# Gates of the first MoE split by halves of the tokens, its second chunk's sums prepared inside the first chunk, and the first places and orders of the second MoE changed

## What is computed

```python
def _attn_ref(q, k, v, tau):                     # 4 x 8 heads, 576 x 64
    scores = scale * q @ k.T
    scores = where(scores >= max(scores) - tau, scores, -1e9)
    return softmax(scores) @ v
def _moe_ref(x, w_a, w_b, w_out):                # x 2304 x 512, w_a and w_b 512 x 1536
    return ((x @ w_a) * (x @ w_b)) @ w_out
def _moe2_ref(x, w_in, w_out, g_ln):             # w_in 512 x 1024
    h = x @ w_in
    solu = h * softmax(h)
    return (layer_norm(solu) * g_ln) @ w_out
```

## Time and profile before

| what | value |
|---|---|
| runs | 976.65, 977.17, 977.37 us; median 977.17 |
| profiled execution | 976.68 us, of which the span from first to last instruction is 974.6 us |
| attention | to about 328 us |
| chunk 0 of the first MoE | about 328 to 378.7 us |
| chunks 1 to 4 | 378.7 to about 757 us, 95.0 us each for the middle ones |
| second MoE | from about 757 us |
| granted TensorE clock | 0.998 of full speed over the span |

### The profile page before, as it was taken

How to read it: one execution, slowest core, us unless ns; L and a number is a source line. 1 busy time by engine, 2 the same in 40 slices (tenths; PEclk the granted TensorE clock), 3 DMA queues, 4 the chain that set the end, 5 groups by cost and what they waited for, 6 DMA issues and landing times.

```text
span 974.6 us, 18670 instructions
## 1 busy us (share of the span) xinstructions
PE 943.8 (97%) x6222; PEld 869.4 (89%) x6222; DVE 779.4 (80%) x1298; ACT 508.6 (52%) x823; POOL 601.4 (62%) x570
## 2 busy tenths in 40 slices
PE   5999999999999998999999999999999999999998
PEld 5999999999998998999899999998899778888886
DVE  6778778887878577787878787877888888888884
ACT  3777777777778645333533443335434743333332
POOL 2777777777778454666576657665777754433320
PEclk9999999999999999999999999999999999999999
DMA  6666667666674564222322231123220200000001
GB/s 176 167 153 164 162 151 169 160 152 161 155 176 112 155 213 131 83 69 67 87 87 66 66 108 65 65 73 143 66 76 13 87 23 22 22 22 22 22 22 43
DMA packets 55683, 96.76 MB, mean 99 GB/s; under 512 B 15576, under 2 KB 24408, under 8 KB 55632
## 3 DMA queue, kind: packets, MB, share of 16 engines
q1 hardware_dynamic: 55632, 96.10, 35.9%
HBM read 58.41 MB, written 5.32 MB: 65 GB/s over the span
## 4 chain that ended last, share of the span: by engine, by line
PE 55%; issue 17%; POOL 13%; DVE 8%; ACT 2%; DMA 2%; SPq 1%; POOLq 0%; DVEq 0%; ACTq 0%
PE PS L1678 12%; PE PS L1640 9%; PE PS L1642 8%; POOL w_raw L739 4%; POOL w_raw L736 3%; PE PS L1837 3%; PE PS L1838 3%; PE PS L1839 3%; POOL w_raw L730 3%; PE PS L1894 3%; PE PS L1896 3%; PE PS L1895 3%; POOL w_raw L738 2%; PE PS L1705 2%; PE PS L1707 2%
## 5 line engine op out<-in xcount | busy, mean ns | idle before, releaser
L664 POOL TENSOR_TENSOR p_lo<-prob,p_hi 128x576 fp32r<-128x576 f32 x144 | 208.6, 1451 | 49.8 <-ACT p_hi L859 47.8
L1705 PE MATMUL PS<-x_parts,w_parts 128*128 128x256 f32 x672 | 191.8, 285 | 8.1 <-DVE g_parts L1332 4.2
L1640 PE MATMUL PS<-ops 128*128 128x288 f32 x642 | 182.1, 305 | 13.8 <-DVE ops L1287 6.5
L1706 PE MATMUL PS<-x_parts,w_parts 128*128 128x256 f32 x672 | 190.8, 284 | 0.0
L1707 PE MATMUL PS<-x_parts,w_parts 128*128 128x256 f32 x672 | 190.8, 284 | 0.0
L1642 PE MATMUL PS<-ops 128*128 128x288 f32 x642 | 177.5, 298 | 0.0
L1207 DVE TENSOR_REDUCE neg_max<-PS 128x1 f32<-128x576 f32 x144 | 108.5, 755 | 59.5 <-PE PS L1642 59.4
L732 POOL TENSOR_TENSOR w_parts<-w_raw,w_parts 128x768 fp32r<-128x768 f32 x48 | 90.8, 1893 | 92.4 <-ACT w_parts L986 92.4
L1640 PEld LDWEIGHTS PS<-ops 128*128 128x128 f32 x642 | 122.5, 191 | 22.7 <-issue 12.0
L1705 PEld LDWEIGHTS PS<-x_parts,w_parts 128*128 128x128 f32 x672 | 129.5, 193 | 12.2 <-DVE g_parts L1332 5.7
L1706 PEld LDWEIGHTS PS<-x_parts,w_parts 128*128 128x128 f32 x672 | 129.5, 193 | 1.8
(11 more groups left out here) (170 smaller groups left out, 2271.1 us busy)
## 6 DMA issues: line engine op xcount, KB each, us to landing
w_raw<-w_ab_dram SPq DMA_DIRECT2D x60, 512.0 KB, 3.3
qk_raw<-qkT_dram SPq DMA_DIRECT2D x32, 288.0 KB, 3.0
ops<-qk_hi SPq DMA_DIRECT2D x62, 144.0 KB
ops<-qk_hi SPq DMA_DIRECT2D x31, 288.0 KB
ops<-qk_lo SPq DMA_DIRECT2D x62, 144.0 KB
v_raw<-v_tiles_dram SPq DMA_DIRECT2D x32, 160.0 KB, 2.7
xT<-head_sb SPq DMA_DIRECT2D x32, 144.0 KB, 3.1
out_dram<-o_sb SPq DMA_DIRECT2D x18, 256.0 KB, 2.0
```

The costliest lines, as they stand in the source:

```text
L664: pool.tensor_tensor(p_lo[:, s, :], prob[:, s, :], p_hi[:, r, :].bitcast(F32), ALU.subtract).then_inc(p_lo_done, 1)
L1640: pe.matmul(ps[:, b, 0:HALF], weights[0][:, r, own], moving[0][:, r, cols], start=(n == 0), stop=False)
L1705: pe.matmul(up_ps(bank, half), w[:, 0, :], x[:, 0, :], start=(k == 0), stop=False)
L1706: pe.matmul(up_ps(bank, half), w[:, 0, :], x[:, 1, :], start=False, stop=False)
```

## The change

- The gates of chunks 1 to 4 are split by halves of the tokens. The first gate is put into the second half of bank 2. ACT makes its high part after number 7, DVE its low part (`low_half`) between numbers 8 and 9. The second half follows after number 9. The next tile's third pair waits for `low_half` alone (at f > 0), its last block for the second half.
- The sums and blocks of x for chunk 1 are split inside tiles 8 to 11 of chunk 0, part 1 first and the first blocks last. The split of the weight sums of tile (1, 0) comes after tile 11. POOL's `prepare(1, 1)` also waits for `low_sums(1, 0)`.
- `high_w(2)` and `low_w(2)` are put ahead of `high_wo(1)`, `low_wo(1)` and the last `invert`.
- In the second MoE `expo_1` and `solu` change places in SBUF. So `solu_step(0, 0)` waits for one `down` less and `expo_step(0, 1)` for one more; the high parts of pair 1 stand ahead of `expo_step(0, 1)`.

```diff
             normed = sb(a, "normed", [P, F2])
+            expo_1 = sb(a, "expo_1", [P, F2])
             solu = sb(a, "solu", [P, F2])
-            expo_1 = sb(a, "expo_1", [P, F2])
...
-        gates_ps = PS[:, 2:4, 0:H]
+        gates_ps = (PS[:, 2, H:2 * H], PS[:, 3, 0:H])
...
                 pool.wait_ge(xs_lo_done, 2 * c)
+                pool.wait_ge(w_sum_lo_done, NF * (c - 1) + 1)
...
                     act.wait_ge(y_done, NF * c + f - 1)
+                act.wait_ge(up_done, UPS * (NF * c + f) + 7)
+                act.activation(half_of(g_part(0, c, f), 0), gates_ps[0], ACT.Copy).then_inc(half_hi_done, 1)
                 act.wait_ge(up_done, UPS * (NF * c + f) + UPS)
-                act.activation(in_halves(g_part(0, c, f)), gates_ps, ACT.Copy).then_inc(g_hi_done, 1)
+                act.activation(half_of(g_part(0, c, f), 1), gates_ps[1], ACT.Copy).then_inc(g_hi_done, 1)
...
             high_wo(0)
+            high_w(2)
             high_wo(1)
-            high_w(2)
             high_wo(2)
...
                 if f == NF - 1:
                     high_x_block(1, 0)
+                high_gate(f)
+
+                if f == NF - 4:
                     high_x_block(1, 1)
-                    high_sums(1, 0)
-                high_gate(f)
+                if f == NF - 3:
+                    high_x_block(1, 2)
+                if f == NF - 2:
+                    high_x_block(1, 3)
                 if f + 2 < NF:
                     high_w(f + 2)
                     high_wo(f + 2)
-            high_x_block(1, 2)
-            high_x_block(1, 3)
             high_blocks(1, 1)
+            high_sums(1, 0)
...
             expo_step(0, 0)
-            high_y(1, (0,))
-            act.wait_ge(y_done, LAST + 10)
+            high_y(1, (0, 1, 2))
+            act.wait_ge(y_done, LAST + 11)
             expo_step(0, 1)
-            high_y(1, (1, 2))
...
+            def low_half(c, f):
+                dve.wait_ge(half_hi_done, NF * (c - 1) + f + 1)
+                dve.tensor_tensor(half_of(g_part(1, c, f), 0), gates_ps[0], half_of(g_part(0, c, f), 0).bitcast(F32),
+                                  ALU.subtract).then_inc(half_lo_done, 1)
...
-                done(dve.tensor_tensor(up_ps(2, 0), first, up_ps(2, 1), ALU.mult))
+                done(dve.tensor_tensor(up_ps(2, 1), first, up_ps(2, 1), ALU.mult))
                 dve.wait_ge(ab_done, n + 1)
                 done(dve.tensor_tensor(up_ps(3, 0), up_ps(3, 0), up_3[:, :], ALU.add))
+                low_half(c, f)
                 dve.wait_ge(up_done, UPS * n + 8)
                 done(dve.tensor_tensor(up_ps(3, 0), second, up_ps(3, 0), ALU.mult))
                 if f == 0:
...
                 if f == NF - 1:
                     low_x_block(1, 0)
-                    low_x_sums(1, 0)
-                    low_sums(1, 0)
                 low_gate(f)
                 if f == 0:
                     low_wo(0)
+                    low_w(2)
+                    invert(last, 1)
                     low_wo(1)
-                    invert(last, 1)
-                if f + 2 < NF:
+                    low_wo(2)
+                if f > 0 and f + 2 < NF:
                     low_w(f + 2)
                     low_wo(f + 2)
-            low_x_sums(1, 1)
-            low_x_block(1, 1)
+                if f == NF - 4:
+                    low_x_sums(1, 0)
+                if f == NF - 3:
+                    low_x_sums(1, 1)
+                if f == NF - 2:
+                    low_x_block(1, 1)
+            low_sums(1, 0)
...
-                    dve.wait_ge(y_done, LAST + 11)
+                    dve.wait_ge(y_done, LAST + 10)
                 solu_step(p, 0)
...
-                pe.wait_ge(g_lo_done, n)
+                if f > 0:
+                    pe.wait_ge(half_lo_done, m)
+                else:
+                    pe.wait_ge(g_lo_done, n)
                 if f == 0:
                     pe.wait_ge(xs_lo_done, 2 * c)
                 block_product(f, 5, 4, 2, 0)
                 block_product(f, 6, 1, 2, 1).then_inc(up_part, 1)
 
+                pe.wait_ge(g_lo_done, n)
                 if f == 0:
                     pe.wait_ge(xb_lo_done, 2 * c)
```

More of the change, by code:

```diff
@@ L254, in build_program, with half_of @@
         UPS = 9
-        gates_ps = PS[:, 2:4, 0:H]
+        gates_ps = (PS[:, 2, H:2 * H], PS[:, 3, 0:H])
         def first_gate_of(f):
             return gate[:, f % 2 * H:(f % 2 + 1) * H]
-        def in_halves(g):
-            return g.rearrange("p (b n) -> p b n", b=2)
+        def half_of(g, half):
+            return g[:, half * H:(half + 1) * H]
         s_ps = PS[:, 0:2, :]
@@ L308, in build_program @@
         w_hi_done = sem("w_hi_done")
+        w_sum_hi_done = sem("w_sum_hi_done")
         w_sum_done = sem("w_sum_done")
@@ L326, in build_program @@
         g_done = sem("g_done")
+        half_hi_done = sem("half_hi_done")
+        half_lo_done = sem("half_lo_done")
         g_hi_done = sem("g_hi_done")
@@ L730, in prepare @@
                 pool.tensor_tensor(b12, b22, b12, ALU.subtract).then_inc(w_sum_done, 1)
-                pool.wait_ge(w_hi_done, NF + 2 * m + 1)
+                pool.wait_ge(w_hi_done, NF + m + 1)
                 pool.tensor_tensor(w_parts[:, f % 2, 1, 0:3, :], w_raw[:, f % RAW, 0:3, :],
@@ L989, in high_sums @@
                 act.wait_ge(w_sum_done, 4 * (NF * (c - 1) + f) + 4)
-                act.activation(w_parts[:, f % 2, 0, 3:7, :], w_raw[:, f % RAW, :, :], ACT.Copy).then_inc(w_hi_done, 1)
+                act.activation(w_parts[:, f % 2, 0, 3:7, :], w_raw[:, f % RAW, :, :], ACT.Copy).then_inc(w_sum_hi_done, 1)
             def copy_product(c, f):
@@ L1328, in low_gate @@
                                   ALU.subtract).then_inc(g_lo_done, 1)
+            def low_half(c, f):
+                dve.wait_ge(half_hi_done, NF * (c - 1) + f + 1)
+                dve.tensor_tensor(half_of(g_part(1, c, f), 0), gates_ps[0], half_of(g_part(0, c, f), 0).bitcast(F32),
+                                  ALU.subtract).then_inc(half_lo_done, 1)
             def low_gates(c, f):
                 dve.wait_ge(g_hi_done, NF * c + f + 1)
-                dve.tensor_tensor(in_halves(g_part(1, c, f)), gates_ps, in_halves(g_part(0, c, f)).bitcast(F32),
+                dve.tensor_tensor(half_of(g_part(1, c, f), 1), gates_ps[1], half_of(g_part(0, c, f), 1).bitcast(F32),
                                   ALU.subtract).then_inc(g_lo_done, 1)
@@ L1340, in low_sums @@
                 m = NF * (c - 1) + f
-                dve.wait_ge(w_hi_done, NF + 2 * m + 2)
+                dve.wait_ge(w_sum_hi_done, m + 1)
                 dve.tensor_tensor(w_parts[:, f % 2, 1, 3:7, :], w_raw[:, f % RAW, :, :],
@@ L1400, in low_x_sums @@
             def low_x_sums(c, part):
-                dve.wait_ge(xb_hi_done, 4 * (c - 1) + 2 + part)
+                dve.wait_ge(xb_hi_done, 4 * (c - 1) + (1 if isinstance(c, int) and c == 1 else 2) + part)
                 dve.tensor_tensor(x_parts[:, 3 + 2 * part:5 + 2 * part, 1, :, :], x_sums[:, 2 * part:2 * part + 2, :, :],
@@ L1407, in low_x_block @@
                 if part == 0:
-                    dve.wait_ge(xb_hi_done, 4 * (c - 1) + 1)
+                    dve.wait_ge(xb_hi_done, 4 * (c - 1) + (4 if isinstance(c, int) and c == 1 else 1))
                     dve.tensor_tensor(x_parts[:, 0:2, 1, :, :], xT[:, :, tokens(c, 0)].rearrange("p (b k) n -> p b k n", b=2),
@@ L1412, in low_x_block @@
                 else:
-                    dve.wait_ge(xb_hi_done, 4 * c)
+                    dve.wait_ge(xb_hi_done, 4 * c - (1 if isinstance(c, int) and c == 1 else 0))
                     dve.tensor_tensor(x_parts[:, 2, 1, :, :], xT[:, 2:4, tokens(c, 1)],
@@ L1715, in up @@
                 if f == 0:
-                    pe.wait_ge(xb_lo_done, 2 * (c - 1) + 1)
+                    pe.wait_ge(xb_lo_done, 2 * (c - 1) + (2 if isinstance(c, int) and c == 1 else 1))
                 block_product(f, 0, 0, 0, 0)
```

## The result

The changed kernel takes 989.56 us (median of 4 runs, 986.40 to 992.11); the kernel before, in the runs beside it, 976.91. The ratio is 1.0124 (95% interval 1.0109 to 1.0140): slower by 12 to 13 us. The profiled execution is the fastest of the four, 986.40 us, with a span 10.0 us longer than before.

A forecast was written before the change was run, and what follows sets the result against it. PE, busy 97% of the span, was taken as the bound, so only late or slow matmuls count. Terms -0.93 + 4.9 + 5.3 - 0.9 - 0.1 + 3.0 = +11.3 on 976.68 gave 988.0, plus 0.5: median 988.5 us, range 979 to 993.

The forecast's parts named there:

- C: Starts of chunks 2 to 4: DVE's wait in tile 0's `low_half` delays `low_sums`, stall 3.44 us; together +5.3 us.
- D: End of chunk 4: gates by halves shorten the stalls at tiles 10 and 11, -0.9 us.
- A: Tile 2 of chunk 0: the reorder makes `low_w(2)` end earlier and removes PE's stall, -0.93 us.
- B: x of chunk 1 inside chunk 0's tiles 8 to 11: stalls of 9.1 in place of 4.24 us, +4.9 us.
- E: Second MoE: earlier `solu_step(0, 0)`, later copies to xT and first `turn`; -0.1 us, bounds -0.6 and +0.3.
- F: PE's clock: falls of 1.5 us each after two of four new long stalls, +3.0 us, bounds 0 and 6.
- R1: Rival, faster: DVE's wait in tile 0 costs nothing, 967 to 969 us; with half the wait 973 to 976; together 0.12.
- R2: Rival, even: tile 0 stalls are about 2 us and the clock holds; within 0.2%, chance 0.04.
- R3: Rival, slower by little: no clock fall, no DVE-POOL collision, x's move at +2; +3, 980 us, chance 0.24.

The follow-up runs named there:

- E1: Changed kernel with tile 0's `low_half` alone moved behind `low_sums(c, 1)`: 974.5 us, ratio 0.9975 to the kernel before.
- E2: Kernel before with the split of the gates by halves alone, tile 0 included: 988.3 us, ratio 1.0121.
- E9: Changed kernel, but ACT makes tile 0's gates ahead of `high_sums(c, 1)` and `high_blocks(c, 2)`: 976.2 us, ratio 0.9990 to the kernel before.
- E5: Changed kernel with POOL's low part of tile 2's blocks held back until `low_sums(c, 1)` is done: 984.2 us, ratio 1.0063 to the kernel before.
- E3: Kernel before with the split of the gates alone, tile 0's first half behind `low_sums(c, 1)`: 973.8 us, ratio 0.9962.
- E7: Kernel before with the reorder at tile 2 of chunk 0 alone: 977.2 us, ratio 1.0007.
- E6: Changed kernel with the first pair of tile 1 computed twice in each of chunks 1 to 4: 986.9 us, ratio 1.0099 to the kernel before.
- E4: Kernel before with x's sums for chunk 1 moved into chunk 0's last tiles alone, gates whole: 978.6 us, ratio 1.0016.
- E11: Same as E10, but with POOL's wait for `low_sums(1, 0)` kept: 972.4 us, ratio 0.9943 to the kernel before.
- E10: E1 with second MoE as before, x's parts for chunk 1 behind tiles 10 and 11's weights, POOL's wait for `low_sums(1, 0)` removed: 975.2 us.

## Why the prediction was right

**Tile 0 (C, +5.3) was the decisive step and right in each part.** From the third pair of tile 2 in one chunk to that in the next (PE's timeline) there were 95.26 us from chunk 3 to 4 before (591.57 to 686.83) and 96.98 after (600.96 to 697.94, no fall of the clock between them): +1.72 where +1.76 was forecast. The stall was forecast as 3.44 us and was 3.48 in chunk 2. E1, E2 and E9 show the cause: it goes with either of the two orders that make it. E5 shows the share of the collision, 0.8 us each.

**Gates at tiles 1 to 11, and D (-0.9).** All stalls at the third pair went, and none came at the last block. From tile 2's third pair of chunk 4 to PE's last `up` matmul it took 70.43 us before and 69.34 after: -1.1. E3 gives -3.4 for the split without tile 0, -3.0 was worked out from the same terms.

**A (-0.93).** `first_up(8)` began 32.93 us after `first_up(1)` before and 32.07 after: -0.86. The attention ahead of it ended 0.4 us later in the execution profiled after; taking that for part of the effect, I expected half of A to be lost in E7, which the trace doesn't bear out. E7's median shows nothing of A, so the term is seen in the trace alone.

**B (+4.9) had the right mechanism and nearly the right size, but not its tie to the clock.** In the changed kernel the stalls were 2.93, none, 0.61, 0.48 and 3.29 us, forecast 2.9, 0.8, 1.3, 0.8 and 3.3: 7.3 in place of 9.1 us. The three in the middle were short because the clock fell 1.3 us after the first one: PE came later to the waits, which ended when DVE was ready. In E1 no fall followed (PE):

```profile
374.55 0.36 PE L1720 MATMUL PS<-x_parts,w_parts 128*128 128x256 f32 x1 [2.63 <-DVE w_parts L1246]
...
379.54 0.39 PE L1828 MATMUL PS<-g_parts,w_od_rolled 128*128 128x256 f32 x1 [0.45 <-DVE g_parts L1336]
...
382.48 0.36 PE L1729 MATMUL PS<-x_parts,w_parts 128*128 128x256 f32 x1 [1.25 <-DVE x_parts L1428]
...
384.47 0.38 PE L1729 MATMUL PS<-x_parts,w_parts 128*128 128x256 f32 x1 [0.33 <-DVE w_parts L1357]
```

The three are 0.61, 1.41 and 0.49 us here. From `first_up(11)` to the second pair of tile (1, 0) it took 9.92 us in E1 and E6, without a fall, and 9.91 or 9.92 in the changed kernel, E4 and E9, with one: this fall cost nothing. With the stalls of E1 in the middle the sum is 2.93 + 0.61 + 1.41 + 0.49 + 3.29 = 8.7, so B is +4.5 and the forecast 0.4 too large. By E4 the move costs 1.3 us even without the gates' wait.

**E (-0.1).** From PE's last `up` matmul to its last matmul there were 213.73 us before and 213.67 after. The delay of the first `turn` by the copies to xT was seen right (0.35 us idle, 789.49 above). That the earlier `solu` gives nothing has a second cause that I had missed, which the timelines of DVE, POOL and ACT after show:

```profile
781.53 1.21 DVE L1559 TENSOR_TENSOR solu<-PS,expo 128x1024 f32<-128x1024 f32 x1
...
788.04 0.21 DVE L1581 TENSOR_SCALAR small<-small 128x1 f32<-128x1 f32 x1 [2.97 <-POOL small L792]
...
786.20 1.29 POOL L797 TENSOR_TENSOR wout_lo_sb<-wout_raw,wout_hi_a 128x512 fp32r<-128x512 f32 x1 [1.41 <-ACT wout_hi_a L1110]
...
787.30 2.04 ACT L966 ACTIVATE xT<-PS 128x512 f32<-128x512 f32 x4
```

POOL's small power operation stands behind `low_wout(3)`, which waits for ACT; DVE waits 2.97 us for it.

**The clock (F, +3.0) had the forecast count and is about +1.9.** The profiled execution has two falls more than before, but not where I had them: the stall at chunk 1 was no longer followed by one, as it was before, and the one behind `first_up(11)` cost nothing, as said. Those in chunks 2 and 3 cost 1.7 us each: there were 98.47 us from chunk 2 to 3 with a fall and 96.98 from chunk 3 to 4 without, and before the second was 0.2 longer. The one of before cost 1.5, so 3.4 less 1.5. I had added 1.5 us for each fall, wherever it came; one that is followed by a wait for another engine can add nothing.

**The sum, and luck.** With these sizes it is -0.86 + 4.5 + 5.2 - 1.1 - 0.1 + 1.9 = +9.5; from `first_up(1)` to PE's last matmul there were 643.00 us before and 652.58 after, +9.6. The forecast had +11.3, and 988.0 for the profiled execution, which took 986.40. For the median I added 0.5, and it lies 3.2 above the profiled one. That 988.5 is within 1.1 us of the median is thus in part luck: two misses of opposite sign.

The other three executions took 3 to 6 us more than the profiled one and have no trace. Their granted clock on record is 0.984 for the longest and 0.993 for the two of 989.5 us, beside 0.994. By an estimate from the falls of the profiled one (three of 3.4 us at half clock make 0.005) the longest had several more, but the two at 989.5 about one more each, less than 2 of their 3.1 us; the rest is open. In the thirteen traces `first_up(1)` began anywhere from 327.5 to 330.8 us, though no kernel here changes the attention, so part of the spread may lie there.

Of the rivals, R1 was false at its own point of decision: L739's counterpart L742 ended at 486.77 while number 7 ended at 485.20. R2 had the stalls behind tile 0 at 2 us, and in chunks 2 to 4 they were 3.42 to 3.50. R3's premises (no fall, no collision) were false too.

## What to carry to other kernels

An operation put into an engine's order earlier brings its wait along, and everything behind it inherits that wait: follow what the awaited engine has in front of the signal, in every place of the loop where the orders differ (here one tile of twelve), before counting the gain. Where two engines exclude each other, letting the less urgent one stand idle until the urgent operation is through can be the faster order (E11 against E10, 2.8 us). Split parts of a change before judging it: this one held a gain of 3 us and a loss of 15. Before adding the price of a slower stretch, look whether the engine waits right behind it: there it may cost nothing.

## What the runs showed of the hardware

The clock's fall isn't set by the length of the stall alone. In the thirteen traces there are 27 stalls of PE of 2.0 to 5.0 us in the MoE part, and with 18 of them the clock fell for 3.4 us or more, during the stall or within 1.4 us after it; none of 1.84 us or less was. At the same place of the program the clock fell in one chunk and not in the next (stalls of 3.50 and 3.42 us in the changed kernel, chunks 3 and 4; 2.06 and 2.08 us in E6, chunks 2 and 3). A sum of such terms has to count them by chance.

What a fall costs depends on what PE meets next: 1.7 us in chunks 2 and 3 of the changed kernel, where PE had work without a wait, and nothing behind `first_up(11)`, where it waited for DVE soon after. In E5 the clock fell there during the stall and stayed down for 6.8 us, and the second pair of tile (1, 0) came 0.7 us later (10.60 us after `first_up(11)`).
